# Route and seam of a two-stage mixture kernel: gate products, first loads and part of the argmax moved

## What is computed

```python
def _attn_ref(r, k, v, w, u):            # 4 batches, 8 heads, 768 positions, 48 wide
    state = zeros((B, H, D, D))
    for t in range(S):
        kt, vt, rt = k[:, :, t], v[:, :, t], r[:, :, t]
        cur = einsum('bhd,bhe->bhde', u[None] * kt, vt)
        y[:, :, t] = einsum('bhd,bhde->bhe', rt, state + cur)
        state = w[None, :, :, None] * state + einsum('bhd,bhe->bhde', kt, vt)

def _moe_ref(x, w_in, w_out):            # x 3072x384, w_in 384x2048, w_out 2048x384
    h = x @ w_in
    return (h - np.tanh(h)) @ w_out

def _moe2_ref(x, expert_emb, tau, w1, w2):   # 8 experts, w1 384x1024, w2 1024x384 each
    xn = x / (norm(x) + 1e-06); en = expert_emb / (norm(expert_emb) + 1e-06)
    logits = xn @ en.T / tau
    expert_idx = np.argmax(logits, axis=1)
    probs = softmax(logits); gate_w = probs[arange(N), expert_idx]
    for e in range(E):
        mask = expert_idx == e
        out[mask] = gate_w[mask, None] * (np.maximum(x[mask] @ w1[e], 0.0) @ w2[e])
```

## Time and profile before

| | us |
|---|---|
| median of 3 runs | 851.17 |
| lowest and highest | 847.74, 852.49 |
| the profiled execution | 848.86 |
| its span, first to last instruction | 847.1 |

### The profile page before, as it was taken

How to read it: one execution, slowest core, us unless ns; L and a number is a source line. 1 busy time by engine, 2 the same in 40 slices (tenths; PEclk the granted TensorE clock), 3 DMA queues, 4 the chain that set the end, 5 groups by cost and what they waited for, 6 DMA issues and landing times. The chain is left out here.

```text
span 847.1 us, 18162 instructions
## 1 busy us (share of the span) xinstructions
PE 819.8 (97%) x5844; PEld 745.2 (88%) x5845; DVE 640.3 (76%) x983; ACT 507.1 (60%) x1057; POOL 217.9 (26%) x239
## 2 busy tenths in 40 slices
PE   8999989999999999999999999789999999999995
PEld 7767768889999999999999998689999999999994
DVE  8979959999998998998998997714546363637552
ACT  5756777767667667667667765215546363636552
POOL 6345524321111111111112331122222223132111
PEclk9999999999999999999999999769999999999998
DMA  9989943225234234224223755479696859693540
GB/s 245 279 255 278 297 131 94 66 80 179 100 106 154 87 109 151 99 87 161 101 100 123 235 188 182 172 244 387 240 332 238 292 203 388 245 362 121 176 160 9
DMA packets 86430, 157.89 MB, mean 186 GB/s; under 512 B 8060, under 2 KB 23566, under 8 KB 86385
## 3 DMA queue, kind: packets, MB, share of 16 engines
q1 hardware_dynamic: 58672, 100.82, 36.5%
q10 hardware_dynamic: 23744, 45.69, 15.0%
q0 software_dynamic: 3968, 10.82, 3.6%
HBM read 117.97 MB, written 40.70 MB: 187 GB/s over the span
## 5 line engine op out<-in xcount | busy, mean ns | idle before, releaser
L1303 POOL TENSOR_TENSOR ew_l<-ew_raw,ew_h 128x512 fp32r<-128x512 f32 x48 | 62.3, 1299 | 272.3 <-DVE poly L1521 268.0
L1227 PE MATMUL y_ps<-wout_h,g_h 128*128 128x392 f32 x384 | 130.8, 341 | 0.4 <-DVE g_l L1512 0.4
L1228 PE MATMUL y_ps<-wout_l,g_h 128*128 128x392 f32 x384 | 130.4, 340 | 0.0
L1229 PE MATMUL y_ps<-wout_h,g_l 128*128 128x392 f32 x384 | 130.3, 339 | 0.0
L1227 PE MATMUL h_ps<-xT_h,win 128*128 (+1 forms) x288 | 113.3, 394 | 1.2 <-DVE diff L1502 0.8
L1229 PE MATMUL h_ps<-xT_h,win 128*128 (+1 forms) x288 | 113.3, 394 | 0.0
L1228 PE MATMUL h_ps<-xT_l,win 128*128 (+1 forms) x288 | 112.8, 392 | 0.0
L1698 DVE SCALAR_TENSOR_TENSOR ex_hT_l<-e_bank,ex_hT_h 128x512 fp32r<-128x512 f32 x48 | 33.2, 691 | 102.8 <-ACT ex_hT_h L1952 88.0
L1853 PE MATMUL e_bank<-ex_xT_h,w_ex 128*128 128x256 f32 x288 | 81.8, 284 | 3.5 <-DVE ex_xT_l L1691 2.9
L1521 DVE COPY_PREDICATED poly<-large,diff 128x512 f32<-128x512 uint8 x96 | 72.0, 750 | 17.5 <-DVE poly L1517 17.5
L1854 PE MATMUL e_bank<-ex_xT_l,w_ex 128*128 128x256 f32 x288 | 81.5, 283 | 0.0
(11 more groups left out here) (244 smaller groups left out, 1994.0 us busy)
## 6 DMA issues: line engine op xcount, KB each, us to landing
w_raw<-in_w ACTq DMA_DIRECT2D x26, 1536.0 KB
ew_raw<-in_w SPq DMA_DIRECT2D x48, 256.0 KB, 2.7
w_h<-ew_h SPq DMA_DIRECT2D x48, 256.0 KB, 2.3
w_l<-ew_l SPq DMA_DIRECT2D x48, 256.0 KB, 2.0
w_ex<-w_h SPq DMA_DIRECT2D x8, 1536.0 KB
w_ex<-w_l SPq DMA_DIRECT2D x8, 1536.0 KB
kv_sb<-in_kv SPq DMA_DIRECT2D x24, 384.0 KB, 5.6
krT_sb<-in_krT SPq DMA_DIRECT2D x44, 192.0 KB, 6.1
```

What stands on the lines that cost most here:

```text
L1227: pe.matmul(out, lh, rh, start=start, stop=False)
L1228: pe.matmul(out, lh, rl, start=False, stop=False)
L1229: return pe.matmul(out, ll, rh, start=False, stop=stop)
L1303: pool.tensor_tensor(ew_l[:, slot, :], raw, ew_h[:, slot, :].bitcast(F32), ALU.subtract).then_inc(ew_l_made, 1)
```

## The change

- The five argmax operations become a function over a range of tiles. Tiles 0 to 19 are done by VectorE in the last feed-forward group, behind slice 12 of 0 to 15; tiles 20 to 23 stay in the route. `top`, `cand`, `pick` and `onehot` move to other memory.
- SyncE loads expert 0's w2 in slice 15 of the last group, once the last hidden product is done, ahead of the last stores of split w2.
- The first half of the gate products moves from the route's end to the head of `experts`, the second half from there to behind unit 0's 72 hidden products. VectorE takes the gates behind unit 0's hidden low halves. The fillers of 10 and 3 in the route become one of 20.
- ScalarE no longer waits for the turned gates before it loads unit 1's w1 and rounds unit 0's tokens. For that the slots are laid out anew: unit slots at blocks 0-1 and 6-7, second weights at 2-3 and 4-5. TensorE waits for the gates to be taken before it transposes unit 1's second tile into their bank.

```diff
--- before.py
+++ after.py
@@ -132,7 +132,7 @@
             w_at = nc.sbuf_base
             win = sbf("win", [P, 2, WIDE * PARTS], F32R)
             w_ex = nc.alloc_sbuf_tensor_at("w_ex", [P, SLOTS * 2 * PARTS * WIDE], F32R, offset=w_at)
-            raw_at = [w_at + 4 * (2 * PARTS * par + 1) * WIDE for par in range(2)] + [w_at + 4 * (SLOTS * 2 - 1) * PARTS * WIDE]
+            raw_at = [w_at + 4 * (6 * par + 1) * WIDE for par in range(2)] + [w_at + 4 * (SLOTS * 2 - 1) * PARTS * WIDE]
             w_raw = [nc.alloc_sbuf_tensor_at(f"w_raw{i}", [P, WIDE if i < 2 else PARTS * WIDE], F32, offset=at)
                      for i, at in enumerate(raw_at)]
             w_logit = sbf("w_logit", [P, KF, E])
@@ -172,14 +172,13 @@
 
 def unit_weights(w, par):
 
-    at = par * 2 * PARTS * WIDE
+    at = par * 6 * WIDE
     return w[:, at:at + WIDE], w[:, at + WIDE:at + 2 * WIDE]
 
 
 def second_weights(w):
 
-    slots = w[:, 0:2 * 2 * PARTS * WIDE].rearrange("p (s f) -> p s f", s=2)
-    return slots[:, :, 2 * WIDE:].rearrange("p s (h f) -> p s h f", h=2)
+    return w[:, 2 * WIDE:6 * WIDE].rearrange("p (s h f) -> p s h f", s=2, h=2)
 
 
 def load_second(eng, w, w2_h, w2_l, w_loaded, e):
@@ -908,10 +907,11 @@
         spare_q = quad[:, :, :].rearrange("p a f -> p (a f)")
         spare_h = xT_h[:, :]
         spare_l = xT_l[:, :]
-        top = part_of(spare, [P, NT])
-        cand = part_of(spare, [P, NT, E])
-        pick = part_of(spare, [P, NT])
-        onehot = part_of(spare, [P, E, NT])
+        spare_x = xt_sb[:, 1:B, :, :].rearrange("p b q t -> p (b q t)")
+        top = part_of(spare_x, [P, NT])
+        cand = part_of(spare_x, [P, NT, E])
+        pick = part_of(spare_x, [P, NT])
+        onehot = part_of(spare_x, [P, E, NT])
         incl = part_of(spare, [P, E, NT])
         below = part_of(spare, [P, NT, E])
         ex = part_of(spare_q, [P, NT, E])
@@ -957,10 +957,11 @@
         gate_ps = bank7[:, 0:2 * COLS]
         GROUP = 8
         PART = NT // 2
+        KNOWN = NT - B
 
         r_dve = sem("r_dve")
-        tied = sem("tied")
         hot = sem("hot")
+        found = sem("found")
         ranked = sem("ranked")
         summed = sem("summed")
         counted = sem("counted")
@@ -998,7 +999,7 @@
 
         def route_tensor(pe):
             keep_warm(pe, h_ps[1], ident, 8)
-            pe.wait_ge(hot, 1)
+            pe.wait_ge(hot, 2)
             flat = onehot[:, :, :].rearrange("p e n -> p (e n)")
             sums = incl[:, :, :].rearrange("p e n -> p (e n)")
             pe.matmul(rank_ps, lower[:, :], flat, start=True, stop=False)
@@ -1011,16 +1012,34 @@
                 pe.wait_ge(slot_hot, n // GROUP + 1)
                 last = pe.matmul(id_ps, oh_slot[:, n, :], rhs_id[:, n, :], start=(n == 0), stop=(n == NT - 1))
             last.then_inc(ids_turned, 1)
-            keep_warm(pe, h_ps[1], ident, 10)
-            pe.wait_ge(gates_placed, 2)
-            turn_gates(pe, 0)
-            keep_warm(pe, h_ps[1], ident, 3)
+            keep_warm(pe, h_ps[1], ident, 20)
 
         def turn_gates(pe, first):
+            pe.wait_ge(gates_placed, 2 * (first // PART + 1))
             for n in range(first, first + PART):
                 last = pe.matmul(gate_ps, oh_slot[:, n, :], rhs_gate[:, n, :, :].rearrange("p a s -> p (a s)"),
                                  start=(n == 0), stop=(n == NT - 1))
             return last
+
+        def argmax(dve, start, stop):
+
+            n = stop - start
+            passed = 0 if start == 0 else 4
+            own, best = logits[:, start:stop, :], top[:, start:stop]
+            marked, chosen = cand[:, start:stop, :], pick[:, start:stop]
+            dve.tensor_reduce(best, own, AX.X, ALU.max).then_inc(found, 1)
+            dve.wait_ge(found, passed + 1)
+            dve.tensor_tensor(marked, own, best.unsqueeze(2).to_broadcast([P, n, E]), ALU.is_equal).then_inc(found, 1)
+            dve.wait_ge(found, passed + 2)
+            dve.scalar_tensor_tensor(out=marked, in0=marked, scalar=-float(E),
+                                     in1=iota_e[:, :].unsqueeze(1).to_broadcast([P, n, E]),
+                                     op0=ALU.mult, op1=ALU.add).then_inc(found, 1)
+            dve.wait_ge(found, passed + 3)
+            dve.tensor_reduce(chosen, marked, AX.X, ALU.min).then_inc(found, 1)
+            dve.wait_ge(found, passed + 4)
+            dve.tensor_tensor(onehot[:, :, start:stop].rearrange("p e n -> p n e"), marked,
+                              chosen.unsqueeze(2).to_broadcast([P, n, E]), ALU.is_equal).then_inc(hot, 1)
+
         def route_vector(dve):
             done = [0]
 
@@ -1048,17 +1067,10 @@
                 dve.tensor_tensor(unit_l[:, cols], unit_raw[:, cols], unit_h[:, cols].bitcast(F32),
                                   ALU.subtract).then_inc(w1_split, 1)
 
-            experts_wide = iota_e[:, :].unsqueeze(1).to_broadcast([P, NT, E])
-
             dve.wait_ge(logits_kept, CH)
             dve.wait_ge(ew_l_made, KF + IN_LATE + NPIECE)
-            step(dve.tensor_reduce(top[:, :], logits[:, :, :], AX.X, ALU.max))
-            step(dve.tensor_tensor(cand[:, :, :], logits[:, :, :], wide(top[:, :], E), ALU.is_equal))
-            step(dve.scalar_tensor_tensor(out=cand[:, :, :], in0=cand[:, :, :], scalar=-float(E),
-                                          in1=experts_wide, op0=ALU.mult, op1=ALU.add))
-            step(dve.tensor_reduce(pick[:, :], cand[:, :, :], AX.X, ALU.min))
-            dve.tensor_tensor(by_tile(onehot), cand[:, :, :], wide(pick[:, :], E), ALU.is_equal).then_inc(hot, 1)
-            dve.wait_ge(hot, 1)
+            argmax(dve, KNOWN, NT)
+            dve.wait_ge(hot, 2)
             dve.tensor_tensor_scan(incl[:, :, :].rearrange("p e n -> p (e n)"),
                                    resets[:, :, :].rearrange("p e n -> p (e n)"),
                                    onehot[:, :, :].rearrange("p e n -> p (e n)"), 0.0, ALU.mult,
@@ -1257,6 +1269,12 @@
                         sp.wait_ge(xT_l_made, KD * g + KD)
                         load_group(sp, g + 1)
                     for f in range(KF):
+                        if last and f == KF - 1:
+                            sp.wait_ge(h_done, KF * CH)
+                            for i in range(MADE):
+                                sp.wait_ge(ew_h_stored[i], 16 * (NP // MADE + 2))
+                                sp.wait_ge(ew_l_stored[i], 16 * (NP // MADE + 2))
+                            load_second(sp, w, w2_h, w2_l, w_loaded, 0)
                         for j in pieces_at(g, last, f):
                             if is_first(g):
                                 sp.wait_ge(ew_l_made, j + 1)
@@ -1277,11 +1295,6 @@
                 for b in range(B):
                     sp.wait_ge(x_stored[b], 2 * 16 * (CH + 1))
                 groups(sp, group)
-                sp.wait_ge(h_done, KF * CH)
-                for i in range(MADE):
-                    sp.wait_ge(ew_h_stored[i], 16 * (NP // MADE + 2))
-                    sp.wait_ge(ew_l_stored[i], 16 * (NP // MADE + 2))
-                load_second(sp, w, w2_h, w2_l, w_loaded, 0)
                 store(CH - 1)
                 sp.wait_ge(x2_stored, 16 * NT)
                 for i in range(MADE):
@@ -1532,6 +1545,9 @@
                             split_logit_weights()
                         if not last and f in SPLIT:
                             x_low(g + 1, SPLIT.index(f))
+                        if last and f == KF - 4:
+                            dve.wait_ge(logits_kept, CH - 1)
+                            argmax(dve, 0, KNOWN)
 
                 def split_logit_weights():
                     dve.wait_ge(wl_high, 1)
@@ -1731,6 +1747,8 @@
 
                 def step(u, j, par, k):
                     hidden_low(u)
+                    if is_first(u):
+                        take_gates()
                     if k is not None:
                         solo_x_low(k)
                         weights_low(k, 0)
@@ -1750,7 +1768,6 @@
 
                 for t in range(2):
                     x_low(0, t)
-                take_gates()
                 steps(dve, step)
 
             @block.gpsimd
@@ -1835,6 +1852,8 @@
                 def transpose_tokens(u, j, par):
                     for t in range(2):
                         pe.wait_ge(gathered[2 * par + t], (j + 1) * 16)
+                        if t == 1 and isinstance(u, int) and u == 1:
+                            pe.wait_ge(gates_made, 1)
                         for a in range(KD):
                             last = pe.transpose(turn_bank(u, t)[:, a * P:(a + 1) * P], rows[:, 2 * par + t, a * P:(a + 1) * P],
                                                 ident[:, :])
@@ -1916,6 +1935,8 @@
 
                 def step(u, j, par, k):
                     first(u, par)
+                    if is_first(u):
+                        turn_gates(pe, NT // 2).then_inc(gates_turned, 1)
                     if k is not None:
                         transpose_solo(k)
```

(3 more changed lines are left out.)

## The result

The change made the kernel slower by about half a per cent: 853.95 us median (852.6 to 858.77, 13 runs) against 849.56 (846.77 to 854.21, 13 runs), ratio 1.0052 with a 95% interval of 1.0034 to 1.0069. Forecast were 843.8 us, a range of 839 to 849, and 0.69 for faster. The profiled execution after took 856.08 us with a span of 854.3, 7.2 more than before's span.

| | before | after |
|---|---|---|
| last y product that waits for VectorE, to first expert product | 40.5 | 33.0 |
| first expert product at | 559.74 | 554.68 |
| first expert product to the span's end | 287.4 | 299.6 |

A forecast was written before the change was run, and what follows sets the result against it. TensorE, busy 97%, was taken as the bound, with time to gain only where it waits, at route and seam. Terms -10.0 (first expert product sooner), +1.4, +1.5, -0.6, +1.8 gave -5.9 us: 843.0, leaned to 843.8, range 839.0 to 849.0.

The forecast's parts named there:

- part 5: Behind unit 0's first hidden products: 12 gate products, +1.4 us, then a wait for SyncE's announcement, +1.5 us; +2.9 together.
- part 3: Route: expert 0's second weights issued some 8 us earlier, w1 lands sooner, VectorE's wait for first rounded weights goes; -3.60 us.
- Part 1: Last feed-forward group: argmax of 20 tiles there takes 2.0 us and delays the group's end by 1.45 us (0.9 to 1.7).
- Part 2: Route head: argmax of only 4 tiles left, so the rank product's wait of 0.70 us goes; -0.70 us.
- Part 4: Seam between route and experts: shrinks from 10.6 to 3.4 us; first expert product from 559.74 to 549.7, at full clock.
- my cold rival: Seam: transposes and gate products at half speed, first expert product 1.5 us late at 551.2, total 844.5 us; chance 0.12.
- Part 6: Unit 1's first product: its wait of 0.62 us behind ScalarE's three loads goes; -0.6 us.
- Part 7: After the first hidden products: clock falls again during thin gate products and wait, 3.7 us of work at half speed; +1.8 us.
- expert 1's second weights late: Unit 1's output products: SyncE's load, issued about 561 behind ScalarE's three, stalls up to 3 us; 846.0 us, chance 0.12.
- the worst order: Expert 1's second-weight load served last, behind ScalarE's 4.7 MB: there at 581 to 583, asked for at about 580.
- the likelier case: Expert 1's second-weight load gets an equal share of the queues: there at 577, before products ask at about 580.
- The slower rival: SyncE's issue of expert 1's weights waits for room behind ScalarE's 4.7 MB, holding TensorE 12 us; 853.5 us, chance 0.04.

The follow-up runs named there:

- e2b: The changed kernel, with both halves of the gate products ahead of unit 0's hidden products; 848.16 us, 0.9975 of the kernel before.
- e1b: The changed kernel, but SyncE issues expert 2's second weights only when expert 1's have landed; 852.51 us, 1.0027 of the kernel before.
- e3b: The changed kernel, but SyncE announces expert 0's second weights before waiting for the gates and issuing expert 1's load; 853.37 us, 1.0035 of the kernel before.
- f1: The kernel before, with only the argmax of 20 of 24 tiles moved into the last feed-forward group; 850.80 us, 1.0012 of the kernel before.
- f3: e2b, with SyncE also issuing expert 0's second weights one slice sooner; 846.81 us, 0.9982 of the kernel before.
- f4: The changed kernel, but ScalarE's loads for unit 2 and the first solo tile come behind unit 0's last output scaling; 856.87 us, 1.0091 of the kernel before.
- e4b: The changed kernel, but all 24 tiles' argmax stands in the route as before; 852.81 us, 1.0019 of the kernel before.
- g3: f2 with both the f3 edit (expert 0's weights a slice sooner) and the e1b edit (expert 2's load waits); 843.82 us, 0.9940 of the kernel before.
- g2: f2, but SyncE issues expert 2's load only after expert 1's has landed and been announced; 844.76 us, 0.9956 of the kernel before.
- f2: The changed kernel, with all gate products ahead of unit 0's hidden products and all 24 tiles' argmax in the route; 844.56 us, 0.9956 of the kernel before.
- g1: f2, with SyncE issuing expert 0's second weights one slice sooner; 846.33 us, 0.9969 of the kernel before.

## Why the prediction was wrong, point by point

The step that decided it is what part 5 moved and did not price: the second half of the gate products, behind which SyncE issues expert 1's second weights. The sum held nothing for that load coming late, and the rival that named it had 3 us at most. The runs showed a stall of 7.40 us and 1.9 us of half clock behind it, and e2b, which moves only these products back, took the stall away. The second step is part 3, which gave 1.08 us where 3.60 stood in the sum.

**What bounds the kernel** is where the wrong price came from. I read that TensorE is busy 97% of the span, and concluded that time is to be had wherever TensorE waits. I had the row with a DMA share of 1.04 at 387 GB/s and used it only as a bandwidth. Had I drawn the windows over the seam and the 40 us behind it, they would have shown the full stretch from 562 to 600. The question would then have been when SyncE's load of expert 1 is issued, not when TensorE begins.

**Part 1** (said +1.45, ends 0.9 and 1.7; was 2.45). The mechanism was right, waits of 1.38 and 0.66 at the end of the group. The five operations took 2.9 us instead of 2.0. All of the excess is one of them, which runs beside GpSimd's subtraction, and that one was slower too (1.42 us; its mean is 1.30). First VectorE after, then GpSimd:

```profile
505.87 0.33 DVE L1032 TENSOR_TENSOR xt_sb<-logits,xt_sb 128x160 f32<-128x160 f32 x1
506.23 1.31 DVE L1034 SCALAR_TENSOR_TENSOR xt_sb<-xt_sb,iota_e 128x160 f32<-128x160 f32 x1
507.57 0.32 DVE L1038 TENSOR_REDUCE xt_sb<-xt_sb 128x20 f32<-128x160 f32 x1
```
```profile
505.94 1.42 POOL L1316 TENSOR_TENSOR ew_l<-ew_raw,ew_h 128x512 fp32r<-128x512 f32 x1 [2.91 <-DVE poly L1534]
```

It repeats with the same 1.31 in every variant that has it in the group (after, e1b, e2b, e3b, f1, f3, f4), and is 0.36 for 24 tiles in those that have it in the route, where GpSimd does nothing. I took a duration from a stretch in which its neighbour was idle. That the overlap is the cause is argued from these pairs, not tried alone. Not every overlap costs: the operation at 505.87 also reads two tiles in on-chip memory, overlapped the same subtraction for 0.26 us, and took 0.33, where it takes 0.36 for all 24 tiles in the route. The Trainium skill, "GPSIMD Engine Reference", section "Specifications", says that GpSimd shares its SBUF interfaces with VectorE and contends with VectorE instructions that have two SBUF inputs. This operation has two, and its 1.31 us fit that; the 0.33 us ahead of it do not.

**Part 2** (-0.70) held. The rank product came 1.59 later than before with the group's end 2.45 later, -0.86.

**Part 3** (-3.60) gave 1.08: the wait of VectorE is 2.52.

```profile
540.39 2.36 DVE L1067 TENSOR_TENSOR w_ex<-w_raw,w_ex 128x1024 fp32r<-128x1024 f32 x2 [2.52 <-ACT w_ex L996]
```

Two steps failed. The load was issued at 518.45, less than 3 us sooner than the 521.30 of before and not 8: ahead of it in SyncE's program stands the store of piece 14, and its low half is made by GpSimd only at 516.48 to 517.76. And w1 took 9.2 us, not 6, since it shared the time with those 3.1 MB: a slice sooner (f3) it took 7.3, and the wait was gone.

**Part 4** (549.7; was 554.68). VectorE's last gate operation ended at 549.32 instead of 546.3, which is mostly parts 1 and 3. The filler took 6.1 us and ended at 546.05, as said. The barrier took 1.6 us from VectorE's end where I had written 0.5: in all variants whose block ends with VectorE it took 1.5 to 1.7, against 0.49 in before and 0.45 in f1, where TensorE came last. What it waits for there, VectorE's completion or GpSimd's gather (whose issue ends at 548.27), stays open, since both moved together in every run. And the seam was cold. The clock fell to half at 539.5 as before, came back at 543 during the filler, and fell again at 549.5 in the idle 4.90 us, so transposes and gate products ran at half speed (2.75 us for 12), as in my cold rival, at a price of about 0.8 us instead of its 1.5.

**Part 5** held in its two terms: 1.42 and 1.28 against 1.4 and 1.5. **Part 6** held too.

**Part 7** (+1.8) did not come: the granted clock stayed at 1.00 from 560 to 590. But the clock fell in the stall, from 590.5 on, and its 1.9 us came there. The fall at 539.5 that I took for a pattern is in ten of the thirteen profiled executions, during or just behind the row products; in e4b, f1 and g3 the clock stayed at 1.00 there and fell only in the idle time that followed.

**The rivals.** The cause was among them, at 0.12: expert 1's second weights late. I had its place right and its price wrong, 3 us at most against 7.40, and added no clock. (The range's upper end does not follow from its own words either: 846.0 and the whole 2.3 to the median are 848.3, not 849.0.) Three terms were mis-sized. I had the load issued at 561 and it was 566.85, since everything ahead of it came later. I counted 7.8 MB on the wire for the worst order, and 9.7 went through from 566.8 to 593.4 (4.76 for ScalarE, 3.57 for SyncE, of them 0.4 of the next load, 1.38 for GpSimd, which I had left out). And I took an equal share of the queues for the likelier case. The Trainium skill, "DMA: Bandwidth & Descriptors", section "Queues, rings and completion order", has each DMA engine go round the queues packet by packet; in e1b, ScalarE's queue moved 2.42 MB in the first 12 us and SyncE's 1.25. The measurement decides: a third, not a half. What makes the shares uneven was not tried.

The slower rival, an issue that waits for room, was priced on the wrong engine. It exists: f4's 6.82, g2's 6.73. It hit ScalarE, which came second, at a time when SyncE's 3.1 MB or its own pair were already on the way. In after SyncE's issues lasted 0.40 and 0.54. A sign of it stood in the trace of before, where I had seen no pair over 2.11 us: SyncE's stores of x, 0.2 MB each, right behind its own 3.1 MB.

```profile
522.43 3.96 SPq L1237 DMA_DIRECT2D x_dram<-x_sb  x4
```

One of the four took 2.09 us to issue, where the median of the 24 such stores is 0.33.

**The arithmetic of the miss.** I said -5.9 for an execution like the profiled one and it was +7.2, 13.1 off. Up to the first product 5.0 (part 1 1.0, part 3 2.5, the barrier 1.1, the cold seam 0.8, the rest small and of both signs). Behind it 8.1 (the stall 7.40 and its clock 1.9, the first products 0.75, less the 1.8 of part 7 that did not come).

## What to carry to other kernels

Before a change pulls work forward on the busiest engine, draw the DMA share over the 40 us that follow. Where it is full, the bytes set the pace, and the question is which loads are issued sooner; here a signal moved behind 10 us of products held back one load and left the DMA engines idle for 6 us, and that took back more than the whole seam had gained. When work is moved behind other work, ask who waits for the semaphore at its end, and what that engine has to issue. Price an operation where it will run, not where it runs now: next to a busy GpSimd one took 1.31 us instead of 0.36.

## What the runs showed of the hardware

- **How long an issue takes depends on what is under way.** ScalarE's pair of 1.5 MB loads took 1.32 to 1.38 us to issue where its and SyncE's loads went out together after idle DMA engines (after, e1b, e3b, e4b), and 1.21 in f4. Where SyncE's 3.1 MB had been issued before ScalarE's first load, it took 1.65 us at a distance of 7.4 us (g3), 2.53 and 2.54 at 6.6 (f2, g1), 3.38 and 4.04 at 6.2 and 6.1 (f3, e2b), and 6.73 at 3.5 (g2). Before and f1 don't fit that row, with 2.11 and 3.16 at some 13 us; there ScalarE's own load had been issued beside SyncE's. A 0.2 MB store of SyncE's took 2.09 us behind its own 3.1 MB in before, instead of 0.33. What has to be free for an issue was not found out.
- **Queues do not share equally.** With three 1.5 MB loads in ScalarE's queue and two in SyncE's, SyncE's got about a third of the bytes over the first 12 us (e1b: 1.25 MB against 2.42).
- **The clock does not repeat with the same code.** In g2 it held at 1.00 through the seam; in f2, the same code up to there, it fell to 0.50 at 550. Their spans, 843.0 and 842.6, do not differ by it, though g2 has another edit as well.
